# Where the first expert unit's first five products stand between the last steps of a sparse attention

## What is computed

```python
def _attn_ref(q, k, v):                      # q, k, v: 4 x 8 x 576 x 64
    scores = scale * np.matmul(q, k.transpose(0, 1, 3, 2))
    mask_local = (rel >= 0) & (rel < stride)                        # heads 0..3, stride 32
    mask_strided = (rel >= 0) & (pos[None, :] % stride == pos[:, None] % stride)   # heads 4..7
    ...
    return np.matmul(attn, v).astype(np.float32)

def _moe_ref(x, w_gate, w1, w2):             # x: 2304 x 512, w1: 8 x 512 x 1024
    logits = x @ w_gate
    ...                                      # P: exp of the logits, 8 rounds of row and column sums
    for e in range(E):
        h = np.maximum(x @ w1[e], 0.0)
        ye = h @ w2[e]
        out += P[:, e:e + 1] * ye

def _moe2_ref(x, w_in, w_out):               # 512 x 2048, 2048 x 512
    h = x @ w_in
    g = np.where(h > 0.0, h, alpha * (np.exp(np.minimum(h, 0.0)) - 1.0))
    return (g @ w_out)
```

## Time and profile before

| | before |
|---|---|
| median of 3 runs | 2031.73 us (2028.39 to 2032.45) |
| the profiled execution's own time | 2029.9 us |
| its span (first to last instruction) | 2028.1 us |
| PE busy | 2000.2 us (99%) |
| DVE / ACT / POOL busy | 1418.1 / 899.6 / 1161.7 us |
| attention, to the last transposes of its context on PE | up to 151.0 us of the span |

### The profile page before, as it was taken

One profiled execution on the slowest core, in us unless ns is written; L12 is line 12 of the kernel. 1 busy time (PEld: TensorE's weight loads), 2 busy tenths in 40 slices (PEclk: granted clock), 3 DMA queues, 4 the chain that ended last, 5 costly groups with the idle time before them and its releaser, 6 DMA issues. The chain is left out here.

```text
span 2028.1 us, 29832 instructions
## 1 busy us (share of the span) xinstructions
PE 2000.2 (99%) x10621; PEld 1809.1 (89%) x10621; DVE 1418.1 (70%) x2462; ACT 899.6 (44%) x1664; POOL 1161.7 (57%) x1520
## 2 busy tenths in 40 slices
PE   8989999999999999999999999999999999999999
PEld 6879999999999999999999998999999999988998
DVE  5767876666667676666666778776666666778876
ACT  5763343333334333333333577433333333477775
POOL 3447655555555575555555567575555555657663
PEclk9989999999999999999999999999999999999999
DMA  7622212222212122222222212222122222212221
GB/s 137 132 66 84 63 63 74 73 63 65 82 63 63 63 76 71 64 69 77 63 63 74 73 63 63 94 76 71 63 70 76 63 63 74 72 64 63 94 73 52
DMA packets 159299, 147.69 MB, mean 73 GB/s; under 512 B 64432, under 2 KB 126128, under 8 KB 159152
## 3 DMA queue, kind: packets, MB, share of 16 engines
q1 hardware_dynamic: 159152, 145.79, 24.9%
HBM read 141.05 MB, written 4.72 MB: 72 GB/s over the span
## 5 line engine op out<-in xcount | busy, mean ns | idle before, releaser
L536 POOL TENSOR_TENSOR w_lo<-w_raw,w_hi 128x256 fp32r<-128x256 f32 x480 | 354.4, 770 | 719.0 <-ACT w_hi L915 719.0
L770 PE MATMUL psum<-w_hi,h_hi 128*128 128x512 f32 x1440 | 562.0, 390 | 0.6 <-issue 0.6
L772 PE MATMUL psum<-w_hi,h_lo 128*128 128x512 f32 x1440 | 561.8, 390 | 0.0
L771 PE MATMUL psum<-w_lo,h_hi 128*128 128x512 f32 x1440 | 560.3, 389 | 0.0
L1193 DVE SCALAR_TENSOR_TENSOR acc<-psum,prob_eps,acc 128x512 f32<-128x512 f32 x516 | 386.5, 750 | 228.4 <-PE psum L772 218.1
L711 PE MATMUL psum<-x_hi_a,w_hi 128*128 128x384 f32 x1296 | 435.0, 336 | 3.9 <-DVE c L1160 3.1
L714 PE MATMUL psum<-x_hi_a,w_lo 128*128 128x384 f32 x1296 | 434.8, 336 | 0.0
L713 PE MATMUL psum<-x_lo_a,w_hi 128*128 128x384 f32 x1296 | 433.9, 335 | 0.0
L529 POOL TENSOR_TENSOR w_lo<-s_tmp,w_hi 128x256 fp32r<-128x256 f32 x480 | 346.7, 752 | 6.1 <-ACT w_hi L910 6.1
L772 PEld LDWEIGHTS psum<-w_hi,h_lo 128*128 128x128 f32 x1440 | 270.3, 188 | 56.3
L770 PEld LDWEIGHTS psum<-w_hi,h_hi 128*128 128x128 f32 x1440 | 270.3, 188 | 49.8 <-issue 0.9
(11 more groups left out here) (122 smaller groups left out, 2791.0 us busy)
## 6 DMA issues: line engine op xcount, KB each, us to landing
w_raw<-in_moe_w_dram SPq DMA_DIRECT2D x192, 512.0 KB, 3.6
w_raw<-in_moe_w_in_dram SPq DMA_DIRECT2D x24, 512.0 KB, 3.4
w_raw<-in_moe_w_out_dram SPq DMA_DIRECT2D x24, 512.0 KB, 3.7
v_l<-in_v_dram SPq DMA_DIRECT2D x24, 128.0 KB, 2.8
out_dram<-acc SPq DMA_DIRECT2D x2, 1536.0 KB, 6.1
raw_l_q<-in_q_dram SPq DMA_DIRECT2D x8, 288.0 KB, 5.1
raw_l_k<-in_k_dram SPq DMA_DIRECT2D x8, 288.0 KB, 6.2
raw_s_q<-in_q_dram SPq DMA_DIRECT2D x16, 144.0 KB
```

The lines of the kernel that those rows point to most:

```text
L536: pool.tensor_tensor(w2_lo[n % 2][piece], w2_raw[piece], w2_hi[n % 2][piece].bitcast(f32), ALU.subtract).then_inc(w2_lo_s, 1)
L770: pe.matmul(dst, h_hi[:, i, kk, js], w2_hi[s][:, i, :], start=(i == 0), stop=False)
L771: pe.matmul(dst, h_hi[:, i, kk, js], w2_lo[s][:, i, :], start=False, stop=False)
L772: mm = pe.matmul(dst, h_lo[:, i, kk, js], w2_hi[s][:, i, :], start=False, stop=(i == 1))
```

## The change

Three things are changed. First, `p1, p6, p5, p2, p7` of unit 0 stand in steps 10, 11, 12, 13 and 14, one in each, and in the step they stand between the transposes of the exponentials and the context. Second, for unit 0 alone, bank W is bank 5 and bank Z bank 6 (the fills', free by then); X stays bank 1, the odd groups' scores, so that p6 waits for the masks up to group 9. Third, the preparation is put into other steps: splits 2, 3, 4 of `x` one or more steps earlier, the low parts of splits 5 and 6 behind step 13's and 14's normalise, unit 0's weights earlier on POOL, ACT and DVE, and `snap(0)`, `make_u2(0)` and ACT's part of unit 1's weights into steps 11 and 12.

```diff
+        def up_ps(n, acc_bank):
+            if n == 0:
+                acc_bank = {W: FILL, X: X, Z: FILL + 1}[acc_bank]
+            return bank(acc_bank)[:, 0:HTOK]
...
         X0_T = {(2, 5): (1,), (2, 7): (2,), (2, 8): (3,), (3, 0): (4,)}
-        X0_HI = {(2, 5): 0, (2, 9): 1, (3, 0): 2, (3, 2): 3, (3, 4): 4, (3, 6): 5, (3, 8): 6}
-        X0_LO = {(2, 6): 0, (2, 10): 1, (3, 1): 2, (3, 3): 3, (3, 5): 4, (3, 7): 5, (3, 9): 6}
-        W0_S = {(3, 2): 0, (3, 4): 1, (3, 6): 2, (3, 8): 3}
-        W0_LO_S = {(3, 10): (0, 1), (3, GROUPS): (2, 3)}
-        W0_HI_A, W0_HI_S, W0_LO_A = (3, 3), (3, 9), (3, 8)
+        X0_HI = {(2, 5): 0, (2, 9): 1, (2, 10): 2, (3, 1): 3, (3, 3): 4, (3, 5): 5, (3, 7): 6}
+        X0_LO = {(2, 6): 0, (2, 10): 1, (3, 0): 2, (3, 2): 3, (3, 4): 4, (3, GROUPS + 2): 5, (3, GROUPS + 3): 6}
+        W0_S = {(3, 1): 0, (3, 2): 1, (3, 3): 2, (3, 4): 3}
+        W0_LO_S = {(3, 7): (0, 1), (3, 8): (2, 3)}
+        W0_HI_A, W0_HI_S, W0_LO_A = (3, 4), (3, 6), (3, 6)
+
+        P1_AT, P6_AT, P5_AT, P2_AT, P7_AT = [(B - 1, GROUPS + i) for i in range(-1, 4)]
+        SNAP_AT, U2_AT, W1_HI_A = (B - 1, GROUPS), (B - 1, GROUPS + 1), (B - 1, GROUPS + 2)
...
                     transpose_exps(*e)
+                if (b, g) == P1_AT:
+                    p1(0)
+                if (b, g) == P6_AT:
+                    pe.wait_ge(masked, GROUP_ALL - 1)
+                    p6(0)
+                if (b, g) == P5_AT:
+                    p5(0)
+                if (b, g) == P2_AT:
+                    p2(0)
+                if (b, g) == P7_AT:
+                    p7(0)
                 if (e := behind(b, g, LAG_CX)) and e[1] < GROUPS:
                     context(*e)
...
-                if (b, g) == (B - 1, GROUPS):
-                    pe.wait_ge(masked, GROUP_ALL)
-                    p1(0)
-                if (b, g) == (B - 1, GROUPS + 1):
-                    p6(0)
-                if (b, g) == (B - 1, GROUPS + 2):
-                    pe.wait_ge(prob_out, GROUP_ALL)
-                    p5(0)
-            p2(0)
-            p7(0)
             for r in LOGIT_LATE:
                 logit_round(r)
```

More of the change, by code:

```diff
@@ L707, in product @@
                 xh, xl = x_op(n, i)
-                d = bank(dst)[:, 0:HTOK]
+                d = up_ps(n, dst)
                 more = not first
@@ L923, in snap @@
                 wait(act, h_lo_s, 4 * (n - 1) + H21)
-                act.activation(c21[:, :], bank(W)[:, 0:HTOK], ACT.Copy).then_inc(snapped, 1)
+                act.activation(c21[:, :], up_ps(n, W), ACT.Copy).then_inc(snapped, 1)
             def relu_11(n):
@@ L928, in relu_11 @@
                 wait(act, down_done, GT * (n - 1) + HT)
-                act.activation(h_blk(H11), bank(W)[:, 0:HTOK], ACT.Relu).then_inc(h_hi_s, 1)
+                act.activation(h_blk(H11), up_ps(n, W), ACT.Relu).then_inc(h_hi_s, 1)
             def relu_21(n):
@@ L989, in _ @@
                     split_w1_s(0)
+                if (b, g) == SNAP_AT:
+                    snap(0)
+                if (b, g) == W1_HI_A:
+                    split_w1_a(1)
             for u in range(-1, U):
@@ L999, in _ @@
                     elu_r(u, E12, c12[u % 2][:, :])
-                if n < U:
+                if 0 < n < U:
                     snap(n)
@@ L1010, in _ @@
                     elu_e(u, E12)
-                if n + 1 < U:
+                if 0 < n and n + 1 < U:
                     split_w1_a(n + 1)
@@ L1044, in _ @@
                     act.wait_ge(up_done, 7 * n + P2 + 1)
-                    elu_r(n, E11, bank(W)[:, 0:HTOK])
+                    elu_r(n, E11, up_ps(n, W))
                     elu_e(n, E11)
@@ L1140, in make_u2 @@
                 wait(dve, h_lo_s, 4 * (n - 2) + H12)
-                dve.tensor_tensor(c12[n % 2][:, :], bank(X)[:, 0:HTOK], c21[:, :], ALU.add).then_inc(c_made, 1)
+                dve.tensor_tensor(c12[n % 2][:, :], up_ps(n, X), c21[:, :], ALU.add).then_inc(c_made, 1)
             def make_u3(n):
@@ L1145, in make_u3 @@
                 wait(dve, h_lo_s, 4 * (n - 1) + H22)
-                dve.tensor_tensor(c22[:, :], bank(X)[:, 0:HTOK], c21[:, :], ALU.add).then_inc(c_made, 1)
+                dve.tensor_tensor(c22[:, :], up_ps(n, X), c21[:, :], ALU.add).then_inc(c_made, 1)
             def make_c22(n):
                 dve.wait_ge(c_made, 5 * n + U3)
-                dve.tensor_tensor(c22[:, :], bank(Z)[:, 0:HTOK], c22[:, :], ALU.add).then_inc(c_made, 1)
+                dve.tensor_tensor(c22[:, :], up_ps(n, Z), c22[:, :], ALU.add).then_inc(c_made, 1)
             def make_c21(n):
@@ L1154, in make_c21 @@
                 dve.wait_ge(c_made, 5 * n + C22)
-                dve.tensor_tensor(c21[:, :], bank(X)[:, 0:HTOK], c21[:, :], ALU.add).then_inc(c_made, 1)
+                dve.tensor_tensor(c21[:, :], up_ps(n, X), c21[:, :], ALU.add).then_inc(c_made, 1)
             def make_c12(n):
@@ L1239, in _ @@
                     split_w1_a(0)
+                if (b, g) == U2_AT:
+                    make_u2(0)
             for u in range(-1, U):
@@ L1253, in _ @@
                         relu_lo(u, H12, c12[u % 2][:, :])
-                if more:
+                if 0 < n < U:
                     make_u2(n)
@@ L1278, in _ @@
                     if not is_elu(n):
-                        relu_lo(n, H11, bank(W)[:, 0:HTOK])
+                        relu_lo(n, H11, up_ps(n, W))
                     if n > 0 and not late(n):
@@ L1283, in _ @@
                     if is_elu(n):
-                        elu_sum(n, E11, elu[E11][:, :], bank(W)[:, 0:HTOK])
+                        elu_sum(n, E11, elu[E11][:, :], up_ps(n, W))
                 if u >= 0:
```

2 lines of the change are left out of this document (1 added, 1 removed).

## The result

The changed kernel takes 2025.38 us (median of 12 runs, 2023.80 to 2028.26) against 2031.51 us for the kernel before in the same runs (12 runs, 2028.39 to 2034.94). The ratio is 0.9973, with a 95% interval of 0.9965 to 0.9980: 5.5 us faster, between 4.1 and 7.1. The profiled execution spans 2022.0 us, 6.1 less than before.

What follows compares the result with a forecast made beforehand. PE, busy 2000.2 of 2028.1 us, bounds the kernel, with DVE setting the pace at the attention's end. Terms gave 4.4 us, start times 5.0, which was kept: 2031.73 - 5.0 = 2026.7 us, range 2023.7 to 2031.2.

Steps and rivals of the forecast that it cites:

- Up to group 10's scores, nothing gained, 1.7 us idle left: Before step 10: scores at 136.3, 0.1 us late, with some 1.7 us of PE idle between 130.7 and 134.8.
- Steps 10 to 14 without waits: Scores to last context: no PE waits, 2.68 us per step, 9.67 us in all, last context at 145.97 (148.88 before).
- My 1.55 us row: Steps 10 to 14: transposes, context and transposes taken as 1.55 us at full clock, from 146.20 to 147.75.
- Two routes to unit 1, DVE's the later: Last context to unit 1: PE's route gives 153.1, DVE's 153.85, later by 0.7 us, a new wait at `top_to_row`.
- The low splits at 0.94: Before `make_u3`: DVE's low splits 5 and 6 take 0.94 us each with POOL idle; at 1.27 the gain is 4.35.
- Half clock, 2.4 us: From 140 to 146-147: about 6.8 us at 1.2 GHz lose PE some 2.4 us, which the change regains.
- the sum of terms (4.4): Whole gain: 3.36 idle and 2.4 clock go, 1.3 comes, 0.1 is the later start, making 4.4 us.
- the one by start times (5.0): Unit 1's first product moves from 158.87 to 153.85, a gain of 5.0 us, the figure kept.
- The 1.02 us gap: PE's longest idle stretch after 136.17, counted among the many small gaps that made the clock fall.
- that rival: Clock still falls from idle time between 130.7 and 134.8, taking back 2.4 us: gain 2.6, 2029.1 us; 20%.
- POOL as the bound: Rival: POOL's low halves delay both shifts by 4.1 us, half clock returns; 1.5 us slower, 2033.2 us; 5%.
- Each step has a product that waits for nothing, standing where PE used to wait: Steps 10 to 14: masks are ahead and early products fill PE's waits; three steps take 8.04 us.

Runs made afterwards that it cites:

- the two kernels with weights moved: Kernel before with only DVE's split of unit 0's own weights moved ahead of group 7's mask (0.9989), or all unit 0's weight preparation as in the change (0.9987).
- preparation only: The changed kernel with the products back at their old places, without the two waits tied to the old banks; ratio 0.9971.
- both profiles of before: The unchanged kernel before, profiled a second time for comparison with its first profile; nothing changed, median 2031.51 us.
- the old weights: The changed kernel with products at their old places and the five tables of unit 0's weights as before; ratio 0.9990.
- tail only: Kernel before with only `snap`, `make_u2` and ACT's part of unit 1's weights in steps 11 and 12, and the new banks; ratio 0.9989.
- products only: The changed kernel's products, `snap`, `make_u2`, ACT's part of unit 1's weights and banks, with the other preparation as before; ratio 1.0012.
- the two profiles with 3.4 us: The profiles of "tail only" (0.9989) and of the kernel with the old weights (0.9990), each with 3.4 us at half clock.

## Why the prediction was right, and where its reasons were not

The forecast was 5.0 us faster, 2026.7 us in a range of 2023.7 to 2031.2, with 0.58 for faster by over 0.2%. Measured: 5.5 us, 2025.4 us, a tenth of a us beyond the band of 2025.5 to 2027.9 that had 55%. By its own steps:

- *Up to group 10's scores, nothing gained, 1.7 us idle left.* PE's waits there are 1.06 us (0.18, 0.23, 0.32, 0.33), and the scores come 13.68 us after step 4's logits, where it was 13.99 and I had forecast 14.12. DVE's weight split took 1.27 us from start to mask (128.12 to 129.39), not the 1.80 I took over from the earlier trace rows: its second part took 0.41 us, since POOL had no work beside it.
- *Steps 10 to 14 without waits.* Right, and three steps took 2.53, 2.53 and 2.34 us, not 2.68 each; from the scores to the last context it is 9.04 instead of 9.67. My 1.55 us row was measured where the clock was just coming back, which I should have seen in the earlier trace rows. These 0.63 us and the 0.4 of the point above are the difference between 5.0 and 6.05 of distance.
- *Two routes to unit 1, DVE's the later.* From the last context to the end of the largest logits I had 1.53 + 1.88 + 4.35 = 7.76 us; it is 144.38 to 152.14, 7.76. The waits came where they were forecast, 0.38 (0.6) and 0.44 (0.7).
- *The low splits at 0.94.* Two took 1.81 together, beside an idle POOL: the shorter price, as taken.
- *Half clock, 2.4 us.* Too small: less the waits, it is 31.83 us before and 29.16 and 29.11 in the two kernels with weights moved, so 2.7. This is half of the 0.6 us by which the sum of terms (4.4) fell short of the one by start times (5.0). The 1.02 us gap that I counted among the causes begins at 140.37, when the clock has fallen already. Half clock did not come back in the changed kernel, whose waits of steps 8 and 9, 0.32 and 0.33, end 2.3 us apart: that rival's condition, 1.7 us of idle time close together, was not met.
- *POOL as the bound.* The first pair of halves delayed a shift (133.21, at once behind them), the second too (135.57), and no wait on PE came of it.
- *"Each step has a product that waits for nothing, standing where PE used to wait."* This sentence, on which the sum's reasoning rests, is wrong as a cause. With the preparation moved, there is one wait of 0.24 us in steps 10 to 14 to fill; without it, the early products make things worse (39.38 against 34.69). I followed the products because they are what the change is named for, and gave the preparation zero gain since it did not bring group 10's scores forward. Its effect was behind those scores: group 10's mask comes 14.46 us after step 4's logits instead of 17.71, while PE's scores for it come only 0.31 earlier. The working had that mask early too (near 137), and with it what the gain hangs on, but credited the gain to the products. The number is right since it adds up PE's work from the scores on without waits, and that sum is nearly the same for either placement; that the reason given beside it did not spoil it is luck. A sum for "preparation only" beside the forecast might have shown it.

What stays open: the banks were not tried by themselves; they are part of all kernels that have the new `snap` and `make_u2`. Just which pattern of waits makes the clock fall was not settled; each kernel but the one before has one profile.

## To carry to other kernels

When a pipelined stage drains into the next, the order on the engine that feeds it can matter more than where the next stage's first work is slotted in. Here preparation cost nothing behind the last item of the draining stage's critical chain, or far enough ahead for the engine to catch up. It is the amount in front of the last items that counts: two low splits of `x` ahead of groups 8 and 10 were harmless once the rest had moved (30.57), all of it together was not. Before counting a placed piece of work as a gap filler, ask whether the gap survives the rest of the edit, and test the two halves apart. Waits of 0.5 to 1 us on TensorE can cost more than their length: here they brought 6.8 us of half clock, worth 2.5 to 2.8 us, and moving them without removing any, or filling them with useless transposes, gave that back.

## What the runs showed of the hardware

- *The clock falls on short waits.* In both profiles of before it fell behind waits of 0.52 and 0.97 or 0.98 that end 1.6 us apart, for 6.8 us each time; with the old weights it fell behind 1.23 and 1.16, 2.45 apart. In "tail only" it outlasted the same 0.52 and 0.97 and fell behind a third wait, of 1.16. Where 5.04 us of waits lay further apart (the largest three 3.8 and 3.2 us), and where 1.07 and 0.85 were 8 us apart, it stayed at 2.4 GHz. The Trainium skill, "TensorE: Matmul & The Clock Gate", section "A second HAM failure mode: psum-queue depth-cycling", describes such swings from micro-idles between matmul groups; the runs agree. They add that work put into the gaps can pay for itself (2.47 us of distance).
- *Half clock costs 0.39 to 0.47 us per us* in this mix. In three of the five profiles a part of it fell on a wait, where it costs nothing: 1.02 us in the first of before, 0.27 in the second, 1.1 in "products only". Per us in which PE worked it is 0.48 to 0.49 there, near the 0.45 of a product alone (2.06 us against 1.13). For the two profiles with 3.4 us it is 0.45 and 0.39; the base of 29.0 varies by 0.2 us, which is 0.06 in these.
- *A DVE instruction can be held off through two POOL instructions in a row.* In the changed kernel a low split of `x` took 3.05 us on DVE, next to POOL's shift and the sum behind it:

```profile
107.87 3.05 DVE L1122 SCALAR_TENSOR_TENSOR x_lo_a<-t_tmp,x_hi_a 128x768 fp32r<-128x768 f32 x1
```

```profile
107.29 1.04 POOL L487 TENSOR_TENSOR score<-score,neg_max 96x512 f32<-96x512 f32 x1 [3.32 <-DVE neg_max L1092]
108.29 1.81 POOL L513 TENSOR_TENSOR xT<-xT 128x768 f32<-128x768 f32 x1
```

Started at 107.87, it ended 0.82 us behind the second POOL instruction's end at 110.10, and alone it takes 0.95. The same split took 3.04 to 3.06 us in the five other kernels that have it in this place, and 0.95 to 1.28 in those that have it a step later. The Trainium skill, "SBUF — State Buffer", section "Who interferes with whom", has the two shut each other out for a whole instruction; that a waiting DVE is passed over a second time is what these rows add. It cost nothing that shows here, as PE then waited for the values anyway (3.01 us, before 3.12).
